# Strassen's seven block products for the first expert layer, with the token thirds as the outermost loop

## The reference, cut to what matters

```python
logits = x @ w_gate;  P = exp(logits - max)          # 1536 x 8
for _ in range(8):                                    # Sinkhorn
    P /= P.sum(1) + 1e-9;  P /= P.sum(0) + 1e-9;  P *= N / E
for e in range(8):
    h = maximum(x @ w1[e], 0)                         # 1536x512 @ 512x1024
    out += P[:, e:e+1] * (h @ w2[e])                  # 1536x1024 @ 1024x512
```

## Time and profile before

| | us |
|---|---|
| median of three runs | 1465.86 |
| the profiled execution, its own time | 1457.44 |
| its span | 1455.7 |
| attention, from the first scores | 16 to 117 |
| end of attention, first gate | 117 to 131.1 |
| first mixture on PE | 131.1 to 1177.3 |
| second gate, routing, second mixture | 1177.3 to 1455.7 |

### The profile page before, as it was taken

How to read it: one execution, slowest core, us unless ns; L and a number is a source line. 1 busy time by engine, 2 the same in 40 slices (tenths; PEclk the granted TensorE clock), 3 DMA queues, 4 the chain that set the end, 5 groups by cost and what they waited for, 6 DMA issues and landing times.

```text
span 1455.7 us, 18813 instructions
## 1 busy us (share of the span) xinstructions
PE 1403.6 (96%) x7522; PEld 1183.9 (81%) x7522; DVE 530.6 (36%) x1435; ACT 346.1 (24%) x667; POOL 173.1 (12%) x168
## 2 busy tenths in 40 slices
PE   7998999999999999999999999999999975999997
PEld 5886888888888888888888888888888854899997
DVE  5555623233232323233232323233232346887000
ACT  5763211211020211202120211211020211444422
POOL 4540201001010101001010101101010100012111
PEclk9999999999999999999999999999999985999999
DMA  8660201010110101010110101010100023665430
GB/s 189 166 169 32 87 1 58 0 58 0 58 53 5 58 0 58 0 58 0 58 58 0 58 0 58 0 58 1 57 0 0 0 87 127 243 235 189 157 129 23
DMA packets 77266, 94.04 MB, mean 65 GB/s; under 512 B 37280, under 2 KB 43424, under 8 KB 77216
## 3 DMA queue, kind: packets, MB, share of 16 engines
q1 hardware_dynamic: 75168, 87.09, 18.4%
q0 software_dynamic: 2048, 6.29, 1.4%
HBM read 87.08 MB, written 6.29 MB: 64 GB/s over the span
## 4 chain that ended last, share of the span: by engine, by line
PE 90%; DVE 3%; ACT 3%; issue 1%; POOL 1%; DMA 1%; SPq 0%; DVEq 0%; POOLq 0%; ACTq 0%
PE PS L1388 24%; PE PS L1387 24%; PE PS L1389 24%; PE PS L1522 6%; PE PS L1505 5%; PE PS L1331 2%; DVE G L1150 1%; PE PS L1552 1%; PE PS L1312 1%; PE PS L1302 1%; ACT sc L629 1%; PE PS L1469 1%; ACT pt L636 0%; PE PS L1480 0%; PE PS L1488 0%
## 5 line engine op out<-in xcount | busy, mean ns | idle before, releaser
L672 ACT ACTIVATE hhi<-PS 128x512 fp32r<-128x512 f32 x192 | 114.8, 598 | 850.9 <-PE PS L1389 850.9
L1388 PE MATMUL PS<-xlo,w1hi 128*128 128x512 f32 x768 | 299.5, 390 | 0.0
L1387 PE MATMUL PS<-xhi,w1hi 128*128 128x512 f32 x768 | 299.5, 390 | 0.0
L1389 PE MATMUL PS<-xhi,w1lo 128*128 128x512 f32 x768 | 299.4, 390 | 0.0
L1389 PE MATMUL PS<-w2hi,hlo 128*128 128x512 f32 x768 | 298.8, 389 | 0.0
L1387 PE MATMUL PS<-w2hi,hhi 128*128 128x512 f32 x768 | 298.8, 389 | 0.0
L1388 PE MATMUL PS<-w2lo,hhi 128*128 128x512 f32 x768 | 298.8, 389 | 0.0
L957 DVE SCALAR_TENSOR_TENSOR hlo<-PS,hhi 128x512 fp32r<-128x512 f32 x192 | 132.7, 691 | 353.1 <-ACT hhi L672 352.9
L973 DVE SCALAR_TENSOR_TENSOR acc<-PS,prob_e,acc 128x512 f32<-128x512 f32 x180 | 135.1, 751 | 333.4 <-PE PS L1389 333.4
L490 POOL TENSOR_TENSOR w2lo<-raw,w2hi 128x512 fp32r<-128x512 f32 x64 | 81.6, 1307 | 903.8 <-ACT w2hi L569 896.7
L1387 PEld LDWEIGHTS PS<-xhi,w1hi 128*128 128x128 f32 x768 | 144.6, 188 | 30.2
(11 more groups left out here) (221 smaller groups left out, 1114.1 us busy)
## 6 DMA issues: line engine op xcount, KB each, us to landing
raw<-in_w SPq DMA_DIRECT2D x34, 1024.0 KB, 6.1
expert_weights<-in_w SPq DMA_DIRECT2D x10, 2048.0 KB, 11.2
raw<-in_w SPq DMA_DIRECT2D x6, 2048.0 KB, 11.1
vs<-in_v SPq DMA_DIRECT2D x16, 192.0 KB, 3.2
x_rows<-acc SPq DMA_DIRECT2D x3, 1024.0 KB, 8.3
vw<-in_v SPq DMA_DIRECT2D x16, 120.0 KB, 3.1
qs<-in_qT SPq DMA_DIRECT2D x4, 384.0 KB, 4.0
kp<-in_kT SPq DMA_DIRECT2D x4, 384.0 KB, 4.7
```

Of the source, the lines that this page charges most:

```text
L672: act.activation(hhi[:, slot, k, 0:width], PS[:, bank, 0:width], ACT.Relu).then_inc(s_done, 1)
L1387: T.matmul(o, whi, xh, start=first, stop=False)
L1388: T.matmul(o, whi, xl, start=False, stop=False)
L1389: return T.matmul(o, wlo, xh, start=False, stop=last)
```

## The change

x (tokens) and the first weights of a half are cut in quarters, 2 x 2 blocks each: x in 256 columns of D by 256 tokens, w1 in 256 rows by 256 columns. Seven products of blocks (Winograd's form of Strassen) take the place of eight. A product has 2x2x3 = 12 matmuls with 256 moving columns, so `h_products` now has 84 matmuls 128x256 in place of 48 matmuls 128x512. `y_products` keeps its 48.

- **Sums before**: DVE makes four sums of weight quarters for each half (`w1_sums`, in `w1_sum`), and four sums of x quarters for each third (DVE for the first third, POOL `x_sums` for the others). Seven parts of each are split: `w1hi`, `xhi` on ACT (`w1_hi`, `x_hi`), `w1lo`, `xlo` on DVE.
- **Sums after**: the parts use banks 0, 1, 0, 2, 0, 1, 0. A part that doesn't open its bank adds to what stands there. ACT copies the bank after parts 0, 1 and 2 (`part_copy`) into `h_sum`, and DVE adds bank and copy (`h_add`) for three of the four quarters of h. Then `hhi` and `hlo` are made from `h_sum`, the fourth quarter from PSUM. PE waits: part 2 for the copy after part 0, part 4 for that after part 2, part 5 for that after part 1, and part 6 for the second `h_add`.
- **Order of the loops**: thirds of the tokens outermost, then experts, then halves. So the weights are loaded (2 MB a unit of work) and split 48 times, not 16. `w2lo` is made on DVE, not on POOL. x1 of a third is stored when that third is done.
- **Attention**: ACT copies the transposed x once as fp32 (`x_copy`), into `xT0`, which lies in `acc`; DVE no longer makes `xlo` there. `w1_sums` and the seven `w1lo` of the first half stand in the last steps.
- **First gate**: fp32 products in groups of 32 columns, as the second gate (`gate_products(layer, ...)`), then `logit_columns(0)`.

```diff
+            def h_products(i, u, x=None):
+                for n in range(PARTS):
+                    pe.wait_ge(s_w1l, of_unit(i, PARTS, u, n + 1))
+                    if x is not None:
+                        pe.wait_ge(s_xl, PARTS * x + n + 1)
+                    if n == 0 and u:
+                        pe.wait_ge(s_hl, of_unit(i, 4, u, 0))
+                    if n == 2:
+                        pe.wait_ge(s_rc, of_unit(i, 3, u, 1))
+                    if n == 4:
+                        pe.wait_ge(s_rc, of_unit(i, 3, u, 3))
+                    if n == 5:
+                        pe.wait_ge(s_rc, of_unit(i, 3, u, 2))
+                    if n == 6:
+                        pe.wait_ge(s_c, of_unit(i, 3, u, 2))
+                    for f in range(2):
+                        fs = slice(f * P, (f + 1) * P)
+                        for k in range(2):
+                            ins = three(PS[:, PART_BANK[n], f * HC:(f + 1) * HC], w1hi[:, n, k, fs], w1lo[:, n, k, fs],
+                                        xhi[:, n, k, :], xlo[:, n, k, :], PART_OPENS[n] and f == 0 and k == 0, k == 1, True)
+                    ins.then_inc(s_pd, 1)
...
+            def layer1(c, i, last):
+                h_products(i, c * UNITS + 1)
+                y_products(i, c * UNITS)
+                if not last:
+                    h_products(i, c * UNITS + 2)
+                elif c < NC - 1:
+                    h_products(i, c * UNITS + 2, c + 1)
+                y_products(i, c * UNITS + 1)
+
+            h_products(0, 0, 0)
+            for c in range(NC):
+                with pe.Fori(0, E - 1) as i:
+                    layer1(c, i, False)
+                layer1(c, E - 1, True)
...
+            def h_period(i, u, more):
+                if more:
+                    for n in range(SUMS):
+                        w1_sums(i, u + 1, n)
+                        yield
+                h_add(i, u, 0)
+                yield
+                if more:
+                    w1_lo(i, u + 1, 0)
+                    yield
+                h_add(i, u, 1)
+                yield
+                h_lo(i, u, 0)
+                yield
+                h_add(i, u, 2)
+                yield
+                for q in range(1, 4):
+                    h_lo(i, u, q)
+                    yield
+
+            def y_period(i, u, more, x, ys):
+                ys = iter(ys)
+                for n in range(PARTS):
+                    if more and n:
+                        w1_lo(i, u + 1, n)
+                        yield
+                    if x is not None:
+                        x_lo(x, n)
+                        yield
+                    if n in (2, 4, 6):
+                        next(ys, None)
+                        yield
+                for k in range(FC):
+                    w2_lo(i, u, k)
+                    yield
+                for _ in ys:
+                    yield
...
                 ch.step(V.tensor_reduce(red8[:], prob[:].rearrange("p t e -> p e t"), AX.X, ALU.add), f"cs{it}", SINK_AT)
-                if it == 0:
-                    dve.wait_ge(s_hi2, 1)
-                if it < FC:
-                    ins = V.tensor_tensor(w2lo[:, 0, it], raw2[:, 0, it], w2hi[:, 0, it].bitcast(F32), ALU.subtract)
-                if it == FC - 1:
-                    ins.then_inc(s_lo2, 1)
-                h_lo(it, 0, it // FC, it % FC, it % 3, CH, s_hh, s_hl)
+                next(aside, None)
+                next(aside, None)
                 dve.wait_ge(s_par, 2 + it)
```

More of the change, by code:

```diff
@@ L658, in x1T_copies @@
+            def layer1(c, i, last):
+                period(i, c * UNITS + 1, not (last and c == NC - 1), c + 1 if last and c < NC - 1 else None)
+                if not (last and c == NC - 1):
+                    period(i, c * UNITS + 2, True)
+            x_hi(0, 0)
+            act.wait_ge(s_gg, 1)
+            act.copy(group_rows[:], PS[0:GROUP * NC, GROUPS_BANK[0], :]).then_inc(s_ggc, 1)
+            for n in range(1, PARTS):
+                x_hi(0, n)
             def x1T_copies():
@@ L900, in step, with pair @@
                         op0=ALU.add, op1=ALU.min, accum_out=negmax[:, 0:1]).then_inc(f_sc, 1)
-                def pair(i, last):
+                def pair(i, last, first=False):
                     for hp in range(2):
@@ L910, in pair @@
                             dve.wait_ge(f_pv, i * (4 * QT) + (2 * QT * hp + QT * (half + 1) + 1))
+                            if hp == 0 and half == 0 and not first:
+                                dve.wait_ge(s_X, i * NC)
                             x_rows(0, i, hp, half)
-                    for c in range(NC):
-                        x_lo(i, c)
                 qk_lo_first()
-                pair(0, False)
+                pair(0, False, True)
                 with dve.Fori(1, H // 2 - 1) as i:
@@ new lines, in y_products @@
+            def y_products(i, u):
+                pe.wait_ge(s_w2l, of_unit(i, 1, u, 1))
+                pe.wait_ge(s_hl, of_unit(i, 4, u, 4))
+                for k in range(TC):
+                    pe.wait_ge(s_acc, of_unit(i, TC, u, k + 1))
+                    ts = slice(k * P, (k + 1) * P)
+                    for f in range(FC):
+                        ins = three(PS[:, Y_BANKS[k], :], hhi[:, u % 2, f, ts], hlo[:, u % 2, f, ts], w2hi[:, u % 2, f, :],
+                                    w2lo[:, u % 2, f, :], f == 0, f == FC - 1)
+                    ins.then_inc(s_y, 1)
@@ L1378, in x1_logits @@
             def x1_logits(d):
-                for c in range(NC):
-                    pe.wait_ge(s_x1c, d * NC + c + 1)
-                    ins = T.matmul(PS[GROUP * c:GROUP * (c + 1), GROUPS_BANK, :], gate_wide[:, d, :], x1T[:, d, c * CH:(c + 1) * CH],
-                                   start=d == 0, stop=d == DC - 1)
-                return ins
-            def three(o, whi, wlo, xh, xl, first, last):
-                T.matmul(o, whi, xh, start=first, stop=False)
-                T.matmul(o, whi, xl, start=False, stop=False)
-                return T.matmul(o, wlo, xh, start=False, stop=last)
@@ L1420, in _ @@
[L1420 to L1428 removed]
+                pe.wait_ge(s_x1c, (d + 1) * NC)
+                gate_products(1, [d], lambda c, d: x1T[:, d, c * CH:(c + 1) * CH])
             x1_transposes(0)
```

529 lines of the change are left out of this document (290 added, 239 removed).

## The result

The changed kernel takes 1452.11 us (median of four runs, 1451.31 to 1454.47) beside 1464.87 for the kernel before in the same session: ratio 0.9914, 95% interval 0.9896 to 0.9933. It is faster by 12.8 us. The forecast was 27. Measured again in a later session it takes 1445.03 beside 1457.10: 0.9917 (0.9903 to 0.9930). So the direction is right, the time lies in the range given (1427 to 1453), and more than half of the gain is missing.

The account below looks back on a forecast made before the run. PE's matmuls were taken to bound the mixture. Savings of 54.5 (products), 2 (start) and 2 (attention), less 26 (idle) and 6.5 (thirds), made 26; the mixture's end gave 27, hence 1439 us, range 1427 to 1453.

Parts of the forecast that it names:

- I take 0.116, between that and 0.120: Products of h: each 256-column matmul starts 0.116 us after the last, saving 54.5 us over 48 units.
- slower rival: Products of h: the fixed 0.013 us adds to the weight load's 0.112, 0.125 us a matmul, giving 1475; chance 9%.
- A steady unit stays bound by PE: Steady mixture loop: DVE, ACT and loads fit within PE's 20.62 us a unit, so no charge for waits.
- The slack that I had at 0.35 us: Steady unit: the second `h_add` would be ready 0.35 us before part 6 needs it.
- rival of late hand-overs: Steady units: three hand-overs among PE, ACT and DVE each 0.1 us late, 14 us, giving 1453; chance 13%.
- 9 and 6 us ... and one of 6: Mixture start: PE idles 9 us before unit 0's part 6, 6 before unit 1, 6 before its part 6.
- charge of 26 us: Mixture start: PE's idle time in units 0 and 1 costs 26 us.
- my 3 us for them: Mixture start: DVE's operations up to unit 1's second `h_add` take 3 us longer beside POOL's four sums.
- 1.7 us once more, most of it inside: Mixture start: half clock after PE's idling costs 1.7 us once more, mostly within the time already counted.
- Changes of third: At two of 48 units, DVE's seven `xlo` (1.5 us late) and once POOL's sums (3.3 us) cost 6.5 with restarts.
- Attention: 2 us forecast: Attention without DVE's `xlo`: 2 us saved, of 0 to 4, as the next step catches most of it up.
- Tail: From the mixture's end to the kernel's end: unchanged in length, 278 us.

Follow-up runs that it names:

- experiment 2: The changed kernel with every 512-column matmul of y split in two of 256 columns: 1474.13 us, ratio 1.0104 to the kernel before.
- experiment 1: The kernel before with series of 24 matmuls of various widths added on PE ahead of the first mixture; one execution, some 40 us longer.
- experiment 5: The changed kernel with POOL's sums for later thirds started four units later, behind `w2lo` or the last `hlo`: ratios 0.9874 and 0.9858 to the kernel before.
- experiment 4: The changed kernel with one 128x512 DVE operation and its waits put back per transposed chunk in attention: 1456.54 us, ratio 0.9996 to the kernel before.

## Why the prediction was right or wrong

**The failed step is a size: "I take 0.116, between that and 0.120".** It was 0.120. The two bounds were rightly read from the rows: from above "half the columns and the whole 0.013", from below the pace of the rows with 65 columns. Both are real, and the slower of the two sets the distance: 0.120 for the columns, a floor of 0.111 below. There is no middle between two limits of which the larger counts, and half of 0.2267 was a value without a mechanism. The pairs at 0.12 in the earlier trace rows had the answer. 4032 matmuls at 4 ns are 16.1 us, more than the whole miss of 14. The halved y of experiment 2 costs what the 13 ns a matmul say, so it is the width and not the new program around it. The slower rival ("0.112 + 0.013") failed for the same reason: floor and fixed part don't add. The Trainium skill ("TensorE: Matmul & The Clock Gate", LDWEIGHTS) has a load of 128 columns at 107 ns. The floor of 0.111 in experiment 1 agrees within 4 ns. The same page's spacing in the Trainium skill (Back-to-back issue gap), 109 ns for 256 columns, doesn't: 120 here, and the measurement decides.

**A steady unit stays bound by PE: right.** The `h_sum` operations of two units in a row start at 374.84 and 395.81: 20.97 us, and 84 x 0.12 + 48 x 0.2267 is 20.96. DVE at 79% was forecast at 78. The slack that I had at 0.35 us:

```profile
376.27 0.69 DVE L1043 TENSOR_TENSOR h_sum<-PS,h_sum 128x512 f32<-128x512 f32 x1
...
377.42 0.28 PE L1522 MATMUL PS<-xhi,w1hi 128*128 128x256 f32 x1
```

The sum ends at 376.96, part 6 begins at 377.42, without a wait; less 0.12 for the weight load, as I had counted, that is 0.34. The rival of late hand-overs is out: it gave nearly the measured time (1453) for a reason that isn't there.

**The start: the places right, the sum near, its parts off.** "9 and 6 us ... and one of 6" were 7.8, 4.6 and 3.3 at the three places named. y of unit 0 began at 167.45, not 175: h of unit 0 began at 124.64, some 5 us before the 129 to 130 that I had for the logits, the stalls were 5 us shorter, and half clock took part of it back. My own sum had a slip, too: 171.7 and the 1.4 us of part 6 are 173.1, not 174.4, so the charge of 26 us was over 1 us more than its parts. Beside POOL's first sums only DVE operations with two SBUF inputs were slow; my 3 us for them were too many.

```profile
161.87 1.66 DVE L926 TENSOR_TENSOR w_sum<-raw,w_sum 128x512 f32<-128x512 f32 x1
163.45 0.68 DVE L1043 TENSOR_TENSOR h_sum<-PS,h_sum 128x512 f32<-128x512 f32 x1
164.05 1.15 DVE L931 TENSOR_TENSOR w1lo<-raw,w1hi 128x512 fp32r<-128x512 f32 x1
165.12 0.68 DVE L1043 TENSOR_TENSOR h_sum<-PS,h_sum 128x512 f32<-128x512 f32 x1
```

Half clock I had at "1.7 us once more, most of it inside". It was 7.6 us up to 200, in four stretches (from 123.1, 140.1, 150.4 and 167.4), each at or behind idle time of PE. The logits stood at 124.98, not at 129: the attention ended earlier, and x_sum, `xhi` and `xlo` didn't hold them up so long. Even so ACT stood from 118.03 to 122.89 with no release in sight.

```profile
122.89 0.62 ACT L689 CAST xhi<-acc 128x512 fp32r<-128x512 f32 x1 [4.86 <-issue]
```

**Changes of third: 6.5 forecast, 9.4 measured.** DVE's lateness of 1.5 us was 1.4. POOL's 3.3 was 4.0 (5.35 to 1.38 in experiment 5), and the half clock after it, 2.0, was hardly in it. The 0.7 at the end, where PE waits for `w2lo`, I didn't have.

**Attention: 2 us forecast.** It was 5.1 us at the last head against the first profile of the kernel before, 3.8 against the second. "Most of it is caught up in the next step" is wrong, by experiment 4: seven operations with their waits were 4.1 us.

**Tail: right.** Nothing of it belongs to the change.

## What to carry to other kernels

Where two limits bound an instruction, work out both and take the larger; don't split the difference, since an error of 4 ns is 16 us over 4000 matmuls. Cutting a product into fewer columns pays only as far as the fixed part of each matmul allows: here an eighth of h's columns became 7.4% of its time (0.8 of 10.88 us). And where one engine's work bounds a start-up, try several orders, and judge them by the end of the stage, as a stall taken away in one unit came back in the next.

## What the runs showed of the hardware

- An fp32r matmul with its own 128x128 weights costs columns / 2.4 GHz + 13 ns, and not under 111 ns (experiment 1). At half clock the 13 ns don't show: ten starts from 144.54 to 146.46 are 0.213 us apart for 256 columns, which is 256 / 1.2 GHz.
- fp32 without the r at 256 columns starts 0.216 us apart in the series, with two entries for each matmul; bf16 128x128 0.056.
- DVE and POOL took turns where both worked on two SBUF inputs: 1.1 to 1.8 us an operation instead of 0.6, on `w1lo`, `w2lo`, `w_sum` and the `hlo` made from `h_sum`. Operations with a PSUM input kept 0.68 between them. "SBUF — State Buffer" of the Trainium skill (Who interferes with whom) says so of DVE operations with two SBUF inputs beside GpSimd's that read SBUF, and the rows agree.
- PE ran at half clock for 30.7 us in one execution and for 41 us in another while it had no idle time (experiment 4), which I had taken to come only after idling.
